# First heads of attention: the score row of head 0 copied straight from PSUM, head 2's q and k loaded into output buffers, two casts on ScalarE, and another order of work

## The chip, the core and the metric

The kernel runs on one NeuronCore of a Trainium2 chip. The metric is the device time of one execution in microseconds (us), the median of several runs. TensorE (PE) multiplies matrices, VectorE (DVE), ScalarE (ACT) and GpSimd (POOL) do the rest, and SyncE (SP) issues nearly all transfers (DMA) up to the last stage. The engines run on their own and wait for each other by semaphores that only count up.

## The reference

Three stages follow each other. Attention has 4 x 8 = 32 heads of 576 positions and width 64, with a mask in blocks of 64. Its output, 2304 tokens of width 512, goes through a gated MLP, and then each token goes to one of 8 experts.

```python
scores = scale * np.matmul(q, k.transpose(0, 1, 3, 2))
scores = np.where(block_i >= block_j, scores, -1000000000.0)
scores = scores - np.max(scores, axis=-1, keepdims=True)
attn = np.exp(scores)
attn = attn / (np.sum(attn, axis=-1, keepdims=True) + 1e-09)
x = np.matmul(attn, v)                  # 32 heads -> (4, 576, 512)
xk, xr = mix(x, x_prev, mu_k), mix(x, x_prev, mu_r)
x = sigmoid(xr @ w_r) * (np.maximum(xk @ w_k, 0.0) ** 2 @ w_v)
h = np.maximum(x[b, s] @ w1[e], 0.0)    # e: the token's expert, by its gate
out[b, s] = p[e] * (h @ w2[e])
```

## The kernel before

Attention takes one head after another, and the engines work on up to four heads at a time. For one head i the steps are these (the names are those in the code).

- SP loads q and k (`load_qk`, 576 KB) into one of two buffers `qk_raw[i % 2]`. ACT rounds the upper half into `aug` (`cast_tops`). DVE rounds everything into `hi` (`cast_hi`, a CAST of 128x1152) and writes the remainder of q into `aug` (`split_q_lo`). POOL then writes the remainder of k (`split_k`, L531), which waits for `q_split`. A next load into the same buffer waits for all three.
- PE makes rough scores (`head_max`, L707 and L710) in four groups, 0 to 3. DVE takes the negated maximum of each (`head_reduce`, L1380 for groups 0 to 2, L1383 for group 3). Group 3 reuses the banks of groups 0 and 1, so its products wait until DVE has read these.
- PE turns the five columns of maxima into a row (`head_row`, L718), DVE copies it (`copy_row`, L1391), and SP moves it by a transfer (`load_row`) into one partition of `aug`. There it is one row of the operand of the exact scores, so that the maximum is subtracted by the product.
- PE makes the exact scores (`head_scores`, L732 and L733, twelve products in five pieces), ACT takes their exponents (`head_exp`), and PE multiplies them by v. `head_pv_split` (L774 for the early half, L779 for the late) begins only when `row_copied` says that DVE has copied the row of the next head out of the same bank. `head_pv_late` (L787 to L789) adds the rounded part of the late half with the splits that DVE makes (`split_v`, L1483 and L1485, in even heads; `split_p`, L1491). ACT copies the result into `o_raw`, of which there are four buffers (`copy_out`).
- The sums of the exponents go by DMA to DVE (`invert`, L1396) and back, and POOL scales the output (`normalise`, L540).

From head 5 on DVE has one more piece of work in each head, the split of MLP weights (L1415).

The order on each engine is written out by hand. In the loop for head i, PE makes the scores of head i with the groups of `head_max(i + 2)` between them, and the row of head i + 1; DVE goes through this list:

```python
copy_row(i + 1); head_reduce(i + 2, 0); split_v(i // 2)        # split_v in even heads
split_wm_lo(i - 1 - WFIRST); cast_hi(i + NBUF); split_p(i)     # split_wm_lo from head 5
split_q_lo(i + NBUF); head_reduce(i + 2, 1); head_reduce(i + 2, 2)
invert(i - 1); head_reduce(i + 2, 3)
```

Before the loop stand the loads, the mask rows (built by DVE in `aug[0]` and copied to the other two `aug` by the transfers of `copy_masks`, which `aug_copied` counts), and the rough scores of heads 0 and 1.

Of the kernel before, what the change touches and what calls it, by code (L numbers as in the profile page):

```python
# [16 lines left out]
def attention_moe_program(nc, qkT, v, mu_k, mu_r, w_k, w_v, w_r, w_gate9, w1, w2, out):  # L17
# [36 lines left out]
    with ExitStack() as ctx:  # L54
# [258 lines left out]
        h_half, relu_half = sem("h_half"), sem("relu_half")  # L313
        pg_last, last_scaled, last_stored = [sem(n) for n in ("pg_last", "last_scaled", "last_stored")]
# [49 lines left out]
        SLOTS = NHEAD + NBUF  # L364
        out_rows = out.rearrange("b s d -> (b s) d")
# [3 lines left out]
        def _(sp):  # L369
            def load_qk(i):  # L370
                wait(sp, q_split, i - 1)
                wait(sp, k_split, i - 1)
                wait(sp, tops_cast, i - 1)
                sp.dma_start(qk_raw[:, i % 2, :, :],
                             qkT[i:i + 1].rearrange("a d w s -> (a d) w s")).then_inc(qk_loaded[i % 2], 16)
# [7 lines left out]
            def load_row(i):  # L383
# [3 lines left out]
                if i == 0:  # L387
                    sp.wait_ge(aug_copied, 16 * (NBUF - 1))
# [42 lines left out]
            load_qk(0)  # L431
            load_qk(1)
# [14 lines left out]
            for i in range(SLOTS):  # L447
# [6 lines left out]
                if i + 1 < NHEAD:  # L454
                    load_row(i + 1)
                if i + 4 < NHEAD:
                    load_qk(i + 4)
# [54 lines left out]
        def _(pool):  # L512
# [14 lines left out]
            def split_k(i):  # L527
# [3 lines left out]
                nc.gpsimd.tensor_tensor(hi[i % NBUF][DH:P, KEY, :], qk_raw[DH:P, i % 2, 1, :],  # L531
# [158 lines left out]
        def _(pe):  # L690
            mm = nc.tensor.matmul

            def head_max(i, groups):
# [4 lines left out]
                for g in groups:  # L698
                    if g == 0:
                        wait(pe, max_reduced, 4 * i)  # L700
                    if g == 3:
                        pe.wait_ge(max_reduced, 4 * i + 2)
                    for t in ((0, 1), (2,), (3,), (4,))[g]:
# [4 lines left out]
                        else:  # L708
                            for half in range(2):
                                last = mm(ps[0:TAIL, MAXB + half, 0:S // 2], q_tile,  # L710
# [8 lines left out]

            def head_scores(i, pieces):  # L720

                b = i % NBUF
                if pieces[0] == 0:
                    pe.wait_ge(k_split, i + 1)
                    pe.wait_ge(q_split, i + 1)
                    pe.wait_ge(row_loaded[i % 2], 16 * (i // 2) + 16)
# [422 lines left out]
        def _(act):  # L1149
# [19 lines left out]
            def copy_out(i, half):  # L1169
# [3 lines left out]
                if half == 0:  # L1173
                    wait(act, norm_done, i - NOUT + 1)
                nc.scalar.activation(o_raw[:, i % NOUT, q0:q1], ps[:, OUTB + half, 0:q1 - q0], ACT.Identity,
# [10 lines left out]
            def cast_tops(i):  # L1186

                wait(act, scores_t, 5 * (i - NBUF + 1))
                act.wait_ge(qk_loaded[i % 2], 16 * (i // 2) + 16)
                nc.scalar.activation(aug[i % NBUF][0:DH, 0:2 * S].rearrange("p (w s) -> p w s", w=2), qk_raw[0:DH, i % 2, :, :],  # L1190
                                     ACT.Copy).then_inc(tops_cast, 1)

            for i in range(NBUF):
                cast_tops(i)

# [24 lines left out]
            for i in range(NHEAD):  # L1220
                if i:
                    copy_out(i - 1, 1)
                head_exp(i)
# [691 lines left out]
```

## Time and profile before

| what | value |
|---|---|
| median of 3 runs | 771.11 us (770.67 to 771.77) |
| the profiled execution, its own time | 772.05 us |
| its span | 770.3 us |
| PE busy in the span | 741.0 us, 96% |
| DVE busy in the span | 494.1 us, 64% |

The span goes from the first to the last instruction. The share of busy time is a mean over stages: in attention, which ends at about 190 us of the span, DVE is nearly as busy as PE, and later it is not. Times in the rows are us from the span's start. A time line gives start, duration, engine, line, operation and operands, and in brackets how long the engine was idle before and what released it.

### The profile page before, as it was taken

How to read it: one execution, taken by the hardware profiler on the slowest of the kernel's cores; microseconds unless marked ns; L12 is line 12 of the kernel's file. 1: busy time of each engine (PE TensorE's matmuls, PEld its weight loads, DVE VectorE, ACT ScalarE, POOL GpSimd, SP SyncE). 2: the span in 40 equal slices, each digit the busy share in tenths (PEclk: the TensorE clock that was granted, in tenths of full speed). 3: DMA queues.
4: the chain of work that ended last, by engine and by line, in shares of the span. 5: the costliest groups of instructions: out<-in, count | busy, mean ns of one | idle time of the engine just before them, and what ended most of it. 6: DMA issues, size and time to landing. Idle time of an engine off the chain costs nothing.

```text
span 770.3 us, 13475 instructions
## 1 busy us (share of the span) xinstructions
PE 741.0 (96%) x4054; PEld 661.7 (86%) x4055; DVE 494.1 (64%) x905; ACT 357.5 (46%) x702; POOL 182.9 (24%) x215
## 2 busy tenths in 40 slices
PE   5999999998999999999999999999999999999994
PEld 4888888886989999999999998788888788888882
DVE  8899999996586856859487797622223745453261
ACT  4687877875652606244251432222124644353250
POOL 3345455453200000000020000223323232323231
PEclk9999999998999999999999999999999999999997
DMA  5667676551000010100101071167110176441000
GB/s 158 212 202 224 195 228 190 165 159 43 24 1 1 0 42 1 42 1 1 42 1 43 3 270 42 43 246 274 41 32 27 41 257 235 143 144 40 20 22 8
DMA packets 43063, 74.41 MB, mean 97 GB/s; under 512 B 10061, under 2 KB 20470, under 8 KB 43012
## 3 DMA queue, kind: packets, MB, share of 16 engines
q1 hardware_dynamic: 38676, 64.30, 25.3%
q0 software_dynamic: 4336, 9.47, 3.6%
q8 instruction: 27, 0.44, 0.2%
q14 instruction: 24, 0.20, 0.1%
HBM read 65.31 MB, written 10.57 MB: 99 GB/s over the span
## 4 chain that ended last, share of the span: by engine, by line
PE 83%; DVE 10%; issue 2%; ACT 2%; DMA 1%; ACTq 0%; POOL 0%; POOLq 0%; DVEq 0%
PE ps L841 20%; PE ps L842 20%; PE ps L843 20%; PE ps L779 3%; PE ps L707 2%; PE ps L999 2%; PE ps L733 2%; PE ps L732 2%; PE ps L831 2%; DVE negm L1380 2%; PE ps L710 2%; PE ps L774 1%; DVE sig L1564 1%; PE ps L753 1%; PE ps L908 1%
## 5 line engine op out<-in xcount | busy, mean ns | idle before, releaser
L841 PE MATMUL ps<-we_hi,hT_hi 128*128 (+1 forms) x176 | 73.4, 417 | 2.1 <-DVE o_sb L1856 1.4
L841 PE MATMUL ps<-we_hi,xgT_hi 128*128 (+1 forms) x176 | 70.6, 401 | 0.2 <-DVE xgT_lo L1755 0.2
L1317 ACT ACTIVATE hT_hi<-ps 128x512 fp32r<-128x512 f32 x44 | 26.1, 597 | 94.5 <-PE ps L999 49.4
L842 PE MATMUL ps<-we_lo,xgT_hi 128*128 (+1 forms) x176 | 69.7, 396 | 0.0
L843 PE MATMUL ps<-we_hi,xgT_lo 128*128 (+1 forms) x176 | 69.7, 396 | 0.0
L842 PE MATMUL ps<-we_lo,hT_hi 128*128 (+1 forms) x176 | 69.5, 395 | 0.0
L843 PE MATMUL ps<-we_hi,hT_lo 128*128 (+1 forms) x176 | 69.4, 394 | 0.0
L1151 ACT ACTIVATE pT<-ps 128x256 f32<-128x256 f32 (+2 forms) x192 | 63.1, 388 | 9.3 <-PE ps L733 8.9
L841 PE MATMUL ps<-xm_k_hi,wk_hi 128*128 128x384 f32 x192 | 65.2, 339 | 2.0 <-DVE ksq L1543 1.7
L841 PE MATMUL ps<-ksq_hi,wv_hi 128*128 128x384 f32 x192 | 66.0, 344 | 0.9 <-DVE yT L1578 0.9
L531 POOL TENSOR_TENSOR hi<-qk_raw,hi 64x576 fp32r<-64x576 f32 x32 | 45.2, 1412 | 85.8 <-DVE aug L1407 85.8
L842 PE MATMUL ps<-ksq_lo,wv_hi 128*128 128x384 f32 x192 | 64.9, 338 | 0.0
L843 PE MATMUL ps<-ksq_hi,wv_lo 128*128 128x384 f32 x192 | 64.9, 338 | 0.0
L843 PE MATMUL ps<-xm_k_hi,wk_lo 128*128 128x384 f32 x192 | 64.6, 336 | 0.0
L842 PE MATMUL ps<-xm_k_lo,wk_hi 128*128 128x384 f32 x192 | 64.5, 336 | 0.0
L1749 DVE TENSOR_TENSOR we_lo<-we_raw,we_hi (+1 forms) x48 | 55.6, 1221 | 11.3 <-ACT we_hi L1296 11.3
L1564 DVE RECIPROCAL sig<-sig 128x384 f32<-128x384 f32 x24 | 61.3, 2553 | 0.8
L1254 ACT ACTIVATE relu_k<-ps 128x384 f32<-128x384 f32 x48 | 23.6, 491 | 81.2 <-PE ps L843 81.2
L1762 DVE TENSOR_TENSOR hT_lo<-ps,hT_hi 128x512 fp32r<-128x512 f32 x44 | 30.0, 686 | 45.2 <-ACT hT_hi L1317 45.2
L1380 DVE TENSOR_REDUCE negm<-ps 128x1 fp32r<-128x128 f32 (+3 forms) x128 | 56.2, 479 | 2.1 <-PE ps L707 0.3
L732 PE MATMUL ps<-hi 128*128 128x256 f32 (+2 forms) x192 | 53.7, 297 | 2.3 <-ACT pT L1151 2.2
L628 POOL DMA_INDIRECT out<-o_sb,idx_out x21 | 21.5, 1023 | 139.4 <-DVE o_sb L1856 139.4
(277 smaller groups left out, 1835.4 us busy)
## 6 DMA issues: line engine op xcount, KB each, us to landing
we_raw<-w SPq DMA_DIRECT2D x12, 2048.0 KB, 11.8
qk_raw<-qkT SPq DMA_DIRECT2D x32, 576.0 KB, 3.9
v_sb<-v SPq DMA_DIRECT2D x16, 320.0 KB, 4.9
inv<-inv_scratch SPq DMA_DIRECT2D x32, 144.0 KB, 4.3
y_scratch<-ytok SPq DMA_DIRECT2D x6, 768.0 KB, 3.5
wk_raw<-w_k SPq DMA_DIRECT2D x8, 256.0 KB, 4.5
wv_raw<-w_v SPq DMA_DIRECT2D x8, 256.0 KB, 4.9
wr_raw<-w_r SPq DMA_DIRECT2D x4, 256.0 KB, 4.8
```

The source lines that it names most:

```text
L531: nc.gpsimd.tensor_tensor(hi[i % NBUF][DH:P, KEY, :], qk_raw[DH:P, i % 2, 1, :], hi[i % NBUF][DH:P, KEY, :].bitcast(F32), ALU.subtract).th ...
L732: mm(dst, hi[b][:, KEY, keys], hi[b][:, Q, q0:q1], start=True, stop=False)
L841: mm(dst, a_hi, b_hi, start=(k == 0), stop=False)
L842: mm(dst, a_hi, b_lo, start=False, stop=False)
L843: return mm(dst, a_lo, b_hi, start=False, stop=(k == n - 1))
L1151: return nc.scalar.activation(dst, src, ACT.Exp, **kw)
L1254: nc.scalar.activation(relu_k[:, f % 2, :], ps[:, KB + f % 2, 0:NT], ACT.Relu).then_inc(relu_done, 1)
L1317: nc.scalar.activation(hT_hi[:, half * FC // 2:(half + 1) * FC // 2, :].rearrange("p f t -> p (f t)"), ps[:, 3 + half, :], ACT.Copy).then_ ...
L1380: last = vec.tensor_reduce(negm[:, i % 2, t:t + 1], ps[:, bank, col:col + keys], AX.X, ALU.max, negate=True)
L1564: vec.reciprocal(sig[:, d, :], sig[:, d, :]).then_inc(sig_done, 1)
L1749: vec.tensor_tensor(we_lo[part][:, third], we_raw[part][:, third], we_hi[part][:, bass.ds(slot_at(j) + k * EPIECE, EPIECE)].bitcast(F32), ...
L1762: vec.tensor_tensor(hT_lo[:, fs, :].rearrange("p f t -> p (f t)"), ps[:, 3 + half, :], hT_hi[:, fs, :].rearrange("p f t -> p (f t)").bitca ...
```

## The change

It touches heads 0 to 4 only.

- **Row of head 0.** PE makes five products of one row each (`first_row`, 1x128) into one partition, and DVE copies them from PSUM into `aug[0]` (1x512 and 1x128). The transposing product, the copy into `m_rows` and the transfer are gone. The copies wait for `aug_copied`. Group 3 of head 0 goes to banks 0 and 1, so it no longer waits for DVE.
- **Head 2's q and k** go into `o_raw[:, 2:4]`, issued as the third transfer of the program, ahead of v and of the mask copies. Heads 3 and up use the two `qk_raw` buffers in turn, so heads 3 and 4 are loaded once heads 0 and 1 are done with them.
- **Casts.** `cast_hi` of heads 1 and 2 is an ACT instruction (128x1152) right behind `cast_tops`.
- **Order.** Head 0 is taken out of PE's and DVE's loops. PE makes all scores of head 0, the row of head 1, and then the v products with groups 0 to 2 of `head_max(2)` between them; group 3 comes last. DVE reduces all of head 2 and only then makes `cast_hi(3)` and `split_q_lo(3)`.

```diff
 def load_qk(i):
-    wait(sp, q_split, i - 1)          # and k_split, tops_cast
+    before = (0, 0, 0, 1, 2)[i] if i < 5 else i - 1
+    wait(sp, q_split, before)         # and k_split, tops_cast
...
-load_qk(0)
-load_qk(1)
+for i in range(NBUF):
+    load_qk(i)
 load_v(0)
 for b in range(1, NBUF):
     copy_masks(b)
-load_qk(2)
-load_row(0)
 load_qk(3)
+load_qk(4)
+load_row(1)
...
 # TensorE
+def first_row(ts):
+    pe.wait_ge(max_reduced, 3 if ts[0] == 0 else 4)
+    for t in ts:
+        last = mm(ps[0:1, OUTB + t // 4, t % 4 * P:(t % 4 + 1) * P], negm[:, 0, t:t + 1], ident_r[:, :],
+                  start=(t % 4 == 0), stop=(t in (3, 4)))
+    last.then_inc(first_row_out, 1)
...
 head_max(0, (0, 1, 2, 3))
-head_row(0)
+first_row((0, 1, 2, 3))
+first_row((4,))
 pe.wait_ge(aug_copied, 16 * (NBUF - 1))
 head_max(1, (0, 1, 2, 3))
-for i in range(NHEAD):
+head_scores(0, (0, 1, 2, 3, 4))
+head_row(1)
+head_pv_split(0, (0, 1))
+head_max(2, (0, 1, 2))
+head_pv_split(0, (2, 3, 4, 5))
+head_pv_late(0)
+head_max(2, (3,))
+for i in range(1, NHEAD):
...
 # ScalarE
 for i in range(NBUF):
     cast_tops(i)
+    if i:
+        nc.scalar.activation(hi[i][:, :, :], raw_of(i), ACT.Copy).then_inc(hi_cast_act, 1)
...
 # VectorE
-copy_row(0)
-cast_hi(1)
+dve.wait_ge(aug_copied, 16 * (NBUF - 1))
+dve.wait_ge(first_row_out, 1)
+first = aug[0][DH:DH + 1, QLO:QLO + CH * P]
+vec.tensor_copy(first[:, 0:4 * P], ps[0:1, OUTB, :])
+dve.wait_ge(first_row_out, 2)
+vec.tensor_copy(first[:, 4 * P:CH * P], ps[0:1, OUTB + 1, 0:P]).then_inc(row_copied, 1)
 split_q_lo(1)
 for g in range(4):
     head_reduce(1, g)
-cast_hi(2)
-split_q_lo(2)
...
 for i in range(NHEAD):
     if i + 1 < NHEAD:
         copy_row(i + 1)
+    if i == 0:
+        split_q_lo(2)
+        split_v(0)
+        split_p(0)
+        for g in range(4):
+            head_reduce(2, g)
+        cast_hi(NBUF)
+        split_q_lo(NBUF)
+        continue
     if i + 2 < NHEAD:
         head_reduce(i + 2, 0)
```

On DVE, this stood before between the row copy of head 0 and that of head 2 (`hi_72` is head 1's buffer, `hi_68` head 2's, `hi_70` head 3's):

```order
L1391 CAST m_rows<-ps 5x128
L1402 CAST hi_72<-qk_raw 128x1152
L1407 TENSOR_TENSOR aug_73<-qk_raw,hi_72 64x576
L1380 TENSOR_REDUCE negm<-ps 128x1 x4
L1383 TENSOR_REDUCE negm<-ps 64x1
L1402 CAST hi_68<-qk_raw 128x1152
L1407 TENSOR_TENSOR aug_69<-qk_raw,hi_68 64x576
L1391 CAST m_rows<-ps 5x128
L1380 TENSOR_REDUCE negm<-ps 128x1 x2
L1483 CAST v_hi<-v_sb 128x128
```

And this stands in the changed kernel from the row copy of head 1 (first row) to that of head 2 (last row):

```order
L1440 CAST m_rows<-ps 5x128
L1459 TENSOR_TENSOR aug_69<-o_raw,hi_68 64x576
L1537 CAST v_hi<-v_sb 128x128
L1539 TENSOR_TENSOR v_lo<-v_sb,v_hi 128x128
L1545 TENSOR_TENSOR pT_lo<-pT,p_hi 128x320
L1428 TENSOR_REDUCE negm<-ps 128x1 x4
L1432 TENSOR_REDUCE negm<-ps 64x1
L1451 CAST hi_70<-qk_raw 128x1152
L1459 TENSOR_TENSOR aug_71<-qk_raw,hi_70 64x576
L1440 CAST m_rows<-ps 5x128
```

The two casts of heads 1 and 2 are gone from DVE, and head 3's cast and split (`hi_70`, `aug_71`), which stood ahead of the last three reductions of head 2, stand behind all five, directly ahead of head 2's row copy.

On PE, this followed the scores of head 0 before (L774 and L779 are its v products, `aug_69` is head 2):

```order
L707 MATMUL ps<-aug_69 128x384
L774 MATMUL ps<-pT,v_sb 128x256
L774 MATMUL ps<-pT,v_sb 128x128
L707 MATMUL ps<-aug_69 128x512
L779 MATMUL ps<-pT,v_sb 128x320 x2
L779 MATMUL ps<-pT,v_sb 128x192
L779 MATMUL ps<-pT,v_sb 128x64
L710 MATMUL ps<-aug_69 64x288 x2
L787 MATMUL ps<-p_hi,v_hi 128x320
```

And this follows them in the changed kernel:

```order
L738 MATMUL ps<-ident_r,negm 5x128
L805 MATMUL ps<-pT,v_sb 128x256
L805 MATMUL ps<-pT,v_sb 128x128
L727 MATMUL ps<-aug_69 128x128
L727 MATMUL ps<-aug_69 128x256
L727 MATMUL ps<-aug_69 128x384
L727 MATMUL ps<-aug_69 128x512
L810 MATMUL ps<-pT,v_sb 128x320 x2
```

The row of head 1 (the first row) now stands directly ahead of the v products that wait for its copy, and groups 0 and 1 of head 2 have moved behind them; the two 64x288 products of group 3 now follow the last v product.

## Rows read from the trace of the kernel before

**Rows 1.** The page, part 1: busy time of each engine in the span.

```profile
PE 741.0 (96%) x4054; PEld 661.7 (86%) x4055; DVE 494.1 (64%) x905; ACT 357.5 (46%) x702; POOL 182.9 (24%) x215
```

**Rows 2.** One stretch of attention: PE, PEld, DVE, ACT, POOL busy, clock, DMA, GB/s.

```profile
60.00:100.00 40.00, 39.38 (x244) 34.74 (x244) 37.11 (x88) 31.86 (x80) 20.56 (x15) 1.00 0.69 212
```

**Rows 3.** The chain that ended last, 0 to 60 us: start, us, piece.

```profile
13.13 0.21 PE ps L732
...
16.54 0.11 PE ps L733
...
17.13 1.28 PE ps L774 x4
...
18.68 1.57 PE ps L779 x8
20.25 0.27 PE ps L710 x2
...
20.96 0.12 PE ps L732
...
23.19 0.66 PE ps L774 x4
...
26.36 0.12 PE ps L732
```

**Rows 4.** The same chain from 60 to 195 us, its pieces on DVE.

```profile
60.55 0.41 DVE negm L1380
...
71.69 0.42 DVE negm L1380
```

**Rows 5.** Time line of all engines, 0 to 26 us.

```profile
8.31 0.34 SPq L374 DMA_DIRECT2D qk_raw<-qkT  x1
8.49 0.75 DVE L1383 TENSOR_REDUCE negm<-ps 64x1 fp32r<-64x576 f32 x1 [0.24 <-PE ps L710]
...
9.81 0.74 DVE L1402 CAST hi<-qk_raw 128x1152 fp32r<-128x1152 f32 x1
...
10.58 0.75 DVE L1407 TENSOR_TENSOR aug<-qk_raw,hi 64x576 fp32r<-64x576 f32 x1
11.26 1.67 DVE L1380 TENSOR_REDUCE negm<-ps 128x1 fp32r<-128x128 f32 x4
...
12.04 1.16 ACT L1190 ACTIVATE aug<-qk_raw 64x1152 fp32r<-64x1152 f32 x1 [4.73 <-DMA qk_raw<-qkT]
...
15.53 1.40 POOL L531 TENSOR_TENSOR hi<-qk_raw,hi 64x576 fp32r<-64x576 f32 x1 [2.64 <-DVE aug L1407]
...
16.02 1.00 DVE L1483 CAST v_hi<-v_sb 128x128 fp32r<-128x128 f32 x1
...
20.55 0.75 DVE L1383 TENSOR_REDUCE negm<-ps 64x1 fp32r<-64x576 f32 x1 [0.42 <-PE ps L710]
...
21.62 0.28 DVE L1391 CAST m_rows<-ps 5x128 fp32r<-5x128 f32 x1 [0.32 <-PE ps L718]
...
22.97 0.76 DVE L1402 CAST hi<-qk_raw 128x1152 fp32r<-128x1152 f32 x1 [0.38 <-PE ps L733]
```

**Rows 6.** Time line of DVE, 19 to 62 us.

```profile
27.90 0.22 DVE L1483 CAST v_hi<-v_sb 128x128 fp32r<-128x128 f32 x1
...
36.94 0.21 DVE L1396 RECIPROCAL sums<-sums 64x9 f32<-64x9 f32 x1 [0.30 <-DMA sums<-o_raw]
```

**Rows 7.** DVE's groups, 0 to 190 us: busy, mean ns, idle before, its releasers.

```profile
L1402 DVE CAST hi<-qk_raw 128x1152 fp32r<-128x1152 f32 x32 | 24.1, 752 | 0.8 <-PE ps L733 0.8
...
L1391 DVE CAST m_rows<-ps 5x128 fp32r<-5x128 f32 x32 | 8.9, 278 | 10.2 <-PE ps L718 10.2
```

**Rows 8.** Stretches of 1 us: clock, mean share of the 16 DMA engines, GB/s.

```profile
3.00:4.00 1.00, 1.00 0.99 392
...
7.00:8.00 1.00, 1.00 0.28 36
```

**Rows 9.** Waits of SP's queue, 0 to 30 us: what for, total, times, longest.

```profile
SPq L388 <- DMA aug<-aug: 0.6, 1, 0.6
```

More of the change, by code:

```diff
@@ L364, in attention_moe_program, with raw_of, raw_in, rows_in @@
         SLOTS = NHEAD + NBUF
+        def raw_of(i):
+            if i == 2:
+                return o_raw[:, 2:4, :]
+            return qk_raw[:, i if i < 2 else (i - 1) % 2, :, :]
+        def raw_in(i):
+            if i < 2:
+                return qk_loaded[i], 16
+            if i == 2:
+                return qk_loaded_2, 16
+            return qk_loaded[(i - 1) % 2], 16 * ((i + 1) // 2)
+        def rows_in(i):
+            return 16 * ((i + 1) // 2)
         out_rows = out.rearrange("b s d -> (b s) d")
@@ L370, in load_qk @@
             def load_qk(i):
-                wait(sp, q_split, i - 1)
[L372 to L375, printed above, removed]
+                before = (0, 0, 0, 1, 2)[i] if i < 5 else i - 1
+                wait(sp, q_split, before)
+                wait(sp, k_split, before)
+                wait(sp, tops_cast, before)
+                sp.dma_start(raw_of(i), qkT[i:i + 1].rearrange("a d w s -> (a d) w s")).then_inc(raw_in(i)[0], 16)
             def load_v(j):
@@ L453, in _ @@
                     spread_sums(i - 1)
-                if i + 1 < NHEAD:
+                if 1 < i + 1 < NHEAD and i:
                     load_row(i + 1)
-                if i + 4 < NHEAD:
+                if i and i + 4 < NHEAD:
                     load_qk(i + 4)
@@ L700, in head_max @@
                         wait(pe, max_reduced, 4 * i)
-                    if g == 3:
+                    if g == 3 and i:
                         pe.wait_ge(max_reduced, 4 * i + 2)
@@ L709, in head_max @@
                             for half in range(2):
-                                last = mm(ps[0:TAIL, MAXB + half, 0:S // 2], q_tile,
+                                last = mm(ps[0:TAIL, MAXB + half if i else PBANK[half], 0:S // 2], q_tile,
                                           a[:, KHI + half * (S // 2):KHI + (half + 1) * (S // 2)], start=True, stop=True)
@@ L725, in head_scores @@
                     pe.wait_ge(q_split, i + 1)
-                    pe.wait_ge(row_loaded[i % 2], 16 * (i // 2) + 16)
+                    if i:
+                        pe.wait_ge(row_loaded[i % 2], rows_in(i))
+                    else:
+                        pe.wait_ge(row_copied, 1)
                 for j in pieces:
@@ L1375, in head_reduce @@
                 if g == 0:
-                    wait(dve, max_row, i - 1)
+                    wait(dve, max_row, i - 2)
                 for t in ((0, 1), (2,), (3,), (4,))[g]:
```

39 lines of the change are left out of this document (26 added, 13 removed).

## The prediction

> **What bounds the kernel now.** I read four views, from coarse to fine. The page comes first: PE is busy 96% of the span and DVE 64% [rows 1]. The reader is to see that the second figure misleads, since it is a mean over stages. So I took a stretch of attention next: in 40 us there PE is busy 39.38 and DVE 37.11 [rows 2]. Both are full, and neither can make up much time. Third, the chain that ended last. From 13.13 us on it runs on PE alone for a long time; the scores of head 1 begin at 20.96 and those of head 2 at 26.36, so a head costs 5.40 us, all of it PE [rows 3]. Later the chain crosses to DVE once in two heads: its pieces begin at 60.55 and 71.69, which is 11.14 us for a pair, or 5.57 a head [rows 4]. Fourth, what DVE idles for in attention: 10.2 us ahead of the row copies, 0.32 in each of nearly all heads, which is the way from the last reduction over PE's row product back to DVE, and 0.8 us in all ahead of 32 casts, two waits of 0.4 [rows 5, 7]. So DVE's list is a loop without slack too, apart from heads 1 and 3, where those two waits are. What follows: a delay of DVE or PE at head 2 is carried to the end of attention, and every later stage starts from there. The start decides, and I work out when each engine gets to the copy of head 2's row, which DVE begins at 21.62 now [rows 5].
>
> One more thing about the start: TensorE is slow there. The same four v products take 1.28 us at 17.13 and 0.66 at 23.19, and the eight after 18.68 take 1.57 [rows 3], which for 896 columns in four passes is the upper level of 2.4 GHz, while the first is the lower, 1.2 GHz. So the clock rises at about 18.5 us, after the chain has run on PE without a break from 13.13. The column of the granted clock says 1.00 before that as well [rows 8], so the durations are the evidence.
>
> **The change, part by part.**
>
> *Row of head 0.* The last reduction of head 0 ends at 9.24, and the split of head 1, L1407, starts at 10.58, behind the row copy and the cast of head 1 (0.74) [rows 5]. Now the cast is ScalarE's. ACT has 4.73 us idle before 12.04, and a cast of 1152 columns takes it 1.16 [rows 5]: two of these fit, and that the work moves costs nothing. DVE's two new copies: 1x128 about 0.25 (the row copy, 0.28), 1x512 about 0.6, between 0.54 and 0.7 by the reductions of that width, since four of these with 1280 columns take 1.67 [rows 5]. Group 3 starts 0.2 sooner, as its 0.24 of idle time goes [rows 5]. With no other wait DVE would be at L1407 at 9.05 + 0.05 + 0.6 + 0.25 = 9.95, a gain of 0.6.
>
> *But the copies wait for the mask rows.* SP's queue issued at 8.31, was done at 8.65 and then waited 0.6 for `aug_copied`, so these landed at 9.25 [rows 5, 9]. Now 576 KB more stand ahead of them, 1.5 us at 392 GB/s [rows 8]. The DMA engines were only 0.28 busy from 7 to 8 us [rows 8], so the mask copies did not wait for data to the end and some of the 1.5 is absorbed. I take 0.5: landing at 9.8, bounds 9.25 and 10.75. Then the copies end at 10.65 and L1407 starts at 10.6, against 10.58. The gain of 0.6 is gone (bounds: 0.55 gained to 0.9 lost). The transfer removed saves nothing in itself: before, the scores of head 0 at 13.13 came straight behind the rough scores of head 1, not behind a landing.
>
> *PE, head 0.* Scores begin at 13.15. Their twelve products, whose first and last piece are at 13.13 and 16.54, add up to 2.77 us on the chain without the other products between them [rows 3] (3200 columns at 1.2 GHz are 2.67), so they end at 15.9. The row product of head 1 ends at 16.05, DVE copies from 16.25 to 16.53 (0.3 for the way there, 0.28) [rows 5], and the v products, which wait for `row_copied`, begin at 16.57: PE idles 0.5 where it had other work before. Early v products 1.28, to 17.85 [rows 3]. Groups 0 to 2 of head 2 are 1280 columns, 1.07 at the lower level; 0.65 of it before 18.5 and 0.3 behind, to 18.8. Late v products 1.57, to 20.4, and the three behind them 0.44 (from 20.52, where L710 ends, to 20.96) [rows 3], to 20.82. Only now come the products of group 3, which stood at 20.25.
>
> *DVE, head 0 to 2.* From 16.53 it has `split_q_lo(2)` (0.75), the splits of v (0.5) and p (0.5) and the reductions of groups 0 to 2 (1.7, the length of four such ones) [rows 5]: it is done at about 20.0 and then waits for group 3. The reduction started 0.30 after the product (20.55) [rows 3, 5]: now 21.11 to 21.86. Behind it stand now the cast and split of head 3, 0.68 and 0.68 from start to start (9.81, 10.58 less idle, 11.26) [rows 5]. So the row of head 2 is copied at 21.11 + 0.68 + 0.68 + 0.68 = 23.15, not 21.62: **1.53 late**. PE is ahead of that; it has to wait for `row_copied` at its v products of head 1.
>
> *Head 1.* DVE does not have to wait 0.38 for PE ahead of its cast [rows 5], as PE has the scores done by 23.2: -0.38. But that cast meets POOL. `split_k(3)` starts 0.17 behind L1407's end, at 23.4, and runs 1.40 to 24.8; the cast of head 4 wants to start at 24.05. Before, the cast L1483 began at 16.02 under a POOL instruction of 15.53 to 16.93 and took 1.00, and at 27.90 beside no such one 0.22 [rows 5, 6]: 0.77 more with 0.91 of POOL's left. With 0.75 left I take +0.6, bounds 0 and 0.75. The Trainium skill (SBUF — State Buffer, section "SBUF: two separate sides") says that a VectorE copy in a two-port mode and a GpSimd instruction share a port pair by an exclusive lock, and the later one stands still until the earlier is through; the row of 1.00 us agrees, and by the rule the sum would have 0.75 in the place of 0.6. The same lock holds, it says, for VectorE instructions with two SBUF inputs beside a GpSimd one that reads SBUF; by that the splits of v and p of head 0 would stand behind `split_k(2)`, which the idle time ahead of group 3 takes up but for 0.3 at most, and no row here shows that pair.
>
> *Heads 2 to 6.* POOL's split comes 1.9 late with the rest, so the load of head 5's q and k is issued at about 24.9, not 23.0; its cast on DVE stands at 29.7, and the issue-to-use time of 4.8 covers it. At 36.94 DVE waited 0.30 for the sums' transfer [rows 6]; that transfer is itself later with PE's products, so I credit 0.1. The row product of each head had up to 0.2 between the end of the last reduction and PE's arrival; I credit 0.1.
>
> *Sum:* 1.53 - 0.38 + 0.6 - 0.1 - 0.1 = **+1.55 us**. The profiled execution took 772.05 us by its own time and 770.3 in its span, so 773.6 and 771.85; the median shown is 0.94 below it, so 771.11 + 1.55 = 772.7. About 0.2% (1.5 us) is what a measurement of this kernel can tell from no change, and my number lies right at it.
>
> **Rivals.**
>
> - *The row waits little and POOL costs nothing.* Mask rows land at 9.25, POOL does not hold up the cast, and more of the sums' wait is absorbed (0.28): 1.53 - 0.2 - 0.38 - 0.28 - 0.1 = +0.6, so 771.7. For it: engines had DMA time to spare at 7 us. Against: the row of 1.00 us. No change that can be told, 0.20.
> - *The clock rises later.* PE's new idle 0.5 us falls just before the old rise. If that delays the rise until past 21.9, the late v and the three late products (2.0 us at the upper level) and half of the groups take double: +1.9 at group 3, so 1.55 + 1.8 = +3.3, 774.4. For it: before, the rise came only after unbroken work. 0.18. The Trainium skill (TensorE: Matmul & The Clock Gate, "Part 1: The HAM clock gate") has the slow clock as the resting state that activity lifts, at a moment that varies from run to run; the one rise in this trace agrees with the first, and no run here shows the second.
> - *The clock rises earlier,* as PE is now unbroken from 13.15 to 16.05 with scores only. If it rose by 15.1, PE would be at group 3 at about 19.4, 1.4 sooner, and DVE at the row at 21.8: 1.55 - 1.3 = +0.25, 771.4. 0.06.
> - *The other side: the head start is kept.* DVE does two casts fewer (1.5 us) and 0.6 more of copies. If what I call a loop had slack, DVE would catch up, and what would remain is PE's lead. For it to decide, the row of head 2 must not be copied later than 21.1: group 3 would have to be reduced by 19.1, which is before PE, with the same products to make as before and 0.5 of idle time, can get there. Worth at best the 0.6 of DVE's lead plus the 0.75 that L1483 lost to POOL and the 0.38 ahead of the cast: -1.7, 769.4. 0.05.
>
> **How the numbers follow.** The forecast case (head 2's row 1.2 to 1.9 late, POOL's hold in part or whole, together +1.0 to +2.2) has 0.48, of which I put 0.28 above the bound of 1.5 and 0.20 below, because POOL's hold has more room upwards. Slower by over 0.2%: 0.28 + 0.18 (late clock) = 0.46, and 0.01 for the rest. Within 0.2%: 0.20 + 0.20 + 0.06 = 0.46. Faster: 0.05 and 0.02 for what I have not thought of. The range runs from 770.9, below the early clock's 771.4, to 774.5, which holds about half of the late clock's case: it leaves out 0.07 below and 0.09 above.
>
> **What the profile after would show.** The first row's copies on DVE starting at about 9.8, held by DMA, not at 9.05. ACT with its two casts of 128x1152 done by 10.7. Head 0's scores at about 13.1. PE idle 0.5 ahead of the first v product. DVE idle about 1 us ahead of the reduction of group 3 of head 2 at 21.1, then the row copied at about 23.15. The cast of head 4, at 24, stretched to 1.3 us. PE idle about 1 us ahead of group 3 of head 3, released by DVE. From head 3 on the same list as before at a constant distance of about 1.6. Wrong would be: a distance that shrinks over the heads (then there is slack), a rise of the clock elsewhere than at 18.5 (the v products at 16.6 and 18.8 tell), or a start of head 1's scores before 20.5.

## The result: 2.5 us slower, and the profile after

| what | kernel before | changed kernel |
|---|---|---|
| median of 20 runs each | 771.80 us (769.46 to 773.27) | 774.29 us (771.87 to 776.34) |
| ratio, with its 95% interval | | 1.0031 (1.0020 to 1.0042), that is 1.5 to 3.2 us |
| the profiled executions, own time | 772.05 us | 771.90 us |
| head 2's row copied by DVE | 21.62 | 24.61 |
| head 6's row copied | 43.47 | 46.25 |

The change costs 2.5 us. The forecast was 1.55 with a range up to 3.4 above, so the sign and the range held, and the size was too small. In plain times 774.29 lies 0.2 below the upper end of the range, 774.5. The page of the changed kernel differs from [rows 1] by nothing that tells of it:

```profile
PE 740.0 (96%) x4058; PEld 660.7 (86%) x4059; DVE 494.5 (64%) x904; ACT 359.9 (47%) x704; POOL 182.9 (24%) x215
```

The profiled executions of the two kernels even took the same time, though the changed one is 2.8 us behind all through attention. The stretches of 5 us behind attention say why: TensorE's granted clock fell there in the kernel before (first two rows, columns as in [rows 2]), and in the changed kernel it did not (last two rows). A level of 0.50 is 1.2 GHz and 1.00 is 2.4 GHz.

```profile
185.00:190.00 5.00, 4.13 (x13) 3.50 (x14) 1.76 (x5) 2.99 (x10) 0.00 (x0) 0.56 0.14 33
190.00:195.00 5.00, 5.00 (x23) 3.93 (x22) 0.00 (x0) 3.54 (x10) 1.40 (x1) 0.75 0.01 0
```

```profile
185.00:190.00 5.00, 2.83 (x20) 2.30 (x19) 2.98 (x5) 3.16 (x10) 1.39 (x1) 1.00 0.03 4
190.00:195.00 5.00, 5.00 (x29) 4.05 (x28) 1.80 (x6) 4.06 (x11) 1.41 (x1) 1.00 0.15 32
```

Such a fall, at 185 to 190 us, stands in 9 of the 14 traces of this study, of both orders. What 0.56 and 0.75 leave out of twice 5 us is 2.2 + 1.25 = 3.45 us of full speed, of which PE, busy for 9.13 of the 10, lost about 3 (an estimate from these rows). One pair of profiles would have told "no change". The mean granted clock, which is on record for each execution, bears this out. The changed kernel's 20 executions fall into two groups: eight with a mean of 0.996 or more took 771.87 to 772.89 us, and twelve below it 774.08 to 776.34; the profiled one is of the first group and the second fastest of all. The profiled execution of the kernel before (mean 0.991) is slower than its median. So I compare when each engine gets to the same work in attention, and leave the end of the span to the medians.

This is the chain of the changed kernel from 6 to 29 us: start, duration, piece.

```profile
6.06 4.05 DMA aug<-aug
10.13 0.68 DVE aug L1503
...
11.04 0.75 DVE aug L1459
...
13.59 0.21 PE ps L763
...
16.47 0.42 issue
16.89 1.62 PE ps L805 x4
18.51 1.17 PE ps L727 x4
19.68 1.99 PE ps L810 x8
...
22.17 0.28 PE ps L730 x2
22.51 0.64 issue
23.15 0.75 DVE hi L1451
...
25.41 1.47 DVE hi L1451
...
28.46 0.48 PE ps L730 x2
```

A piece called issue is time for which the chain names no releaser: by the time line, at 16.47 it is PE's wait for the row copy and at 22.51 the reduction of group 3 itself. Before, this chain was on PE alone from 13.13 on [rows 3]. Now it comes from the mask rows' transfer, has PE standing still for 0.42 ahead of the first v product (L805), and leaves PE for DVE twice: behind group 3 of head 2 (L730), and for the cast of head 4. (That cast has two rows in the chain: L1451 at 23.15 is head 3's and at 25.41 head 4's.) The time line of the same stretch:

```profile
9.43 1.15 ACT L1239 ACTIVATE hi<-o_raw 128x1152 fp32r<-128x1152 f32 x1
10.13 0.68 DVE L1503 CAST aug<-ps 1x512 fp32r<-1x512 f32 x1 [1.21 <-DMA aug<-aug]
...
16.50 0.28 DVE L1440 CAST m_rows<-ps 5x128 fp32r<-5x128 f32 x1 [2.13 <-PE ps L738]
...
17.61 1.56 POOL L551 TENSOR_TENSOR hi<-o_raw,hi 64x576 fp32r<-64x576 f32 x1 [4.26 <-DVE aug L1459]
17.62 0.29 DVE L1539 TENSOR_TENSOR v_lo<-v_sb,v_hi 128x128 fp32r<-128x128 f32 x1
17.83 1.70 DVE L1545 TENSOR_TENSOR pT_lo<-pT,p_hi 128x320 fp32r<-128x320 f32 x1
...
22.48 0.75 DVE L1432 TENSOR_REDUCE negm<-ps 64x1 fp32r<-64x576 f32 x1 [1.36 <-PE ps L730]
...
24.61 0.27 DVE L1440 CAST m_rows<-ps 5x128 fp32r<-5x128 f32 x1
...
24.85 1.40 POOL L551 TENSOR_TENSOR hi<-qk_raw,hi 64x576 fp32r<-64x576 f32 x1 [2.90 <-DVE aug L1459]
...
25.34 1.54 DVE L1451 CAST hi<-qk_raw 128x1152 fp32r<-128x1152 f32 x1
26.80 0.48 DVE L1545 TENSOR_TENSOR pT_lo<-pT,p_hi 128x320 fp32r<-128x320 f32 x1
...
30.05 0.28 DVE L1440 CAST m_rows<-ps 5x128 fp32r<-5x128 f32 x1 [0.32 <-PE ps L738]
```

Nearly every step of the prediction can be found: the copies held by the masks' transfer, the idle PE, DVE waiting 1.36 for group 3, the row of head 2 copied behind the cast and split of head 3, and the cast of head 4 stretched under POOL's split. The row copies follow those of before by 2.99 (head 2), 3.03, 3.04, and then 2.78 us from head 5 to the end of attention. The chain's pieces on DVE show the same distance in the place of [rows 4]:

```profile
63.34 0.41 DVE negm L1428
...
74.47 0.41 DVE negm L1428
```

Again 11.13 for a pair of heads, now 2.79 later.

### The profile page after: what moved, and what is told of

Its sections match the earlier page's. It is cut to its first block, busy times and chain, and to the rows that moved or that the text cites. A ratio compares the mean times of both kernels' runs of the same rounds, so it can differ in the third digit from the quotient of the medians.

```text
span 770.2 us, 13482 instructions
## 1 busy us (share of the span) xinstructions
PE 740.0 (96%) x4058; PEld 660.7 (86%) x4059; DVE 494.5 (64%) x904; ACT 359.9 (47%) x704; POOL 182.9 (24%) x215
## 4 chain that ended last, share of the span: by engine, by line
PE 83%; DVE 10%; issue 2%; ACT 2%; DMA 1%; ACTq 0%; POOL 0%; POOLq 0%; SPq 0%; DVEq 0%
PE ps L881 20%; PE ps L883 20%; PE ps L882 20%; PE ps L810 3%; PE ps L727 2%; PE ps L1039 2%; PE ps L764 2%; PE ps L763 2%; PE ps L871 2%; DVE negm L1428 2%; PE ps L730 1%; PE ps L805 1%; DVE sig L1627 1%; DVE hi L1451 1%; PE ps L948 1%
## 5 line engine op out<-in xcount | busy, mean ns | idle before, releaser
L551 POOL TENSOR_TENSOR hi<-qk_raw,hi 64x576 fp32r<-64x576 f32 x31 | 43.8, 1411 | 83.0 <-DVE aug L1459 83.0
L648 POOL DMA_INDIRECT out<-o_sb,idx_out x21 | 21.5, 1023 | 139.4 <-DVE o_sb L1919 139.4
```

Of the source, the lines that this page charges most:

```text
L551: nc.gpsimd.tensor_tensor(hi[i % NBUF][DH:P, KEY, :], raw_of(i)[DH:P, 1, :], hi[i % NBUF][DH:P, KEY, :].bitcast(F32), ALU.subtract).then_i ...
```

## The experiments

Thirteen kernels were compared with the kernel before, always on the same chip. Of each I give the ratio, and two moments from its trace: when the clock rose (from where the records of the granted clock begin; the durations agree) and when the rows of heads 2 and 6 were copied. The first four ask for the place of the delay, the next four for the parts, the last four for the clock.

| kernel | clock rises | row of head 2 | row of head 6 | ratio (95% interval) |
|---|---|---|---|---|
| before | 18.37 | 21.62 | 43.47 | 1 |
| changed | 20.41 | 24.61 | 46.25 | 1.0031 (1.0020, 1.0042) |
| masks_first | 19.88 | 24.12 | 45.87 | 1.0039 (1.0025, 1.0053) |
| cast_before_g3 | 21.61 | 24.07 | 45.66 | 1.0035 (1.0022, 1.0048) |
| g3_before_late | 22.96 | 25.39 | 47.01 | 1.0049 (1.0036, 1.0063) |
| before_delay | 19.27 | 23.19 | 44.01 | 1.0008 (0.9993, 1.0022) |
| fill_gap | 19.46 | 23.73 | 45.36 | 1.0029 (1.0019, 1.0040) |
| old_order | 20.98 | 22.91 | 44.82 | 1.0013 (0.9994, 1.0032) |
| row_only | 21.81 | 23.49 | 45.09 | 1.0002 (0.9992, 1.0012) |
| mended | 19.16 | 23.15 | 44.94 | 1.0017 (1.0008, 1.0026) |
| before_warm | 6.46, falls 9.88, 20.12 | 22.32 | 43.94 | 0.9997 (0.9986, 1.0007) |
| after_warm | 5.62, falls 9.04, 22.69 | 25.71 | 47.34 | 1.0014 (1.0000, 1.0029) |
| old_order_warm | 4.53, falls 7.94, 18.18 | 21.49 | 43.43 | 1.0006 (0.9995, 1.0017) |
| before_warmer | 6.22, stays | 20.60 | 42.17 | 0.9978 (0.9964, 0.9992) |

**masks_first: head 2's load behind the mask copies.**

```diff
-            for i in range(NBUF):
-                load_qk(i)
+            load_qk(0)
+            load_qk(1)
...
+            load_qk(2)
```

> The changed kernel with the load of head 2's q and k issued behind v and the mask copies instead of ahead of them. Marks: the landing of the mask rows (10.1 us in the changed kernel, 9.25 before), the copy of head 2's row on VectorE (24.61 against 21.62) and that of head 6's row (46.25 against 43.47). If the load ahead of the masks is what holds up the first copies: masks at 9.3, the first copy of the row at 9.3, scores of head 0 at 12.8 instead of 13.6, and head 6's row at 45.5 to 45.9, less if the clock rises sooner as well. If the mask rows were late for another reason: nothing moves. If only the moment of the clock's rise counts (20.4 us in the changed kernel, 18.4 before): head 6's row moves only as far as that moment does, by half of it or less.

```profile
9.71 0.68 DVE L1504 CAST aug<-ps 1x512 fp32r<-1x512 f32 x1 [0.79 <-DMA aug<-aug]
```

The copies start 0.42 earlier, head 1's row 0.42 and head 2's 0.49. The wait for the masks is real, and it is a small part: 0.38 us at head 6, with a rise of the clock 0.53 earlier, to which the reckoning below puts all but 0.1 of it. The median, 774.16, does not show it. The masks landed at 9.7 and not at 9.3 as expected (9.25 before); what held them for the other 0.4 is not shown.

**cast_before_g3: the cast and split of head 3 ahead of the last reduction of head 2 on DVE.**

```diff
-                    for g in range(4):
+                    for g in range(3):
                         head_reduce(2, g)
                     cast_hi(NBUF)
                     split_q_lo(NBUF)
+                    head_reduce(2, 3)
```

> The changed kernel with one edit on VectorE: the cast and the q split of head 3 stand ahead of the last reduction of head 2 (group 3), in the 1.36 us that it waits there for TensorE. If the order of VectorE's list makes the lateness: head 2's row is copied at 23.5 instead of 24.61, the cast of head 4 no longer meets the GpSimd split of head 3 (0.75 instead of 1.54 us), head 6's row at 45.1 instead of 46.25, and the median about 1.1 us below the changed kernel's. If the late clock is the cause, TensorE is what is waited for, VectorE's order gives nothing: head 6's row at 46.2.

```profile
20.91 0.74 DVE L1451 CAST hi<-qk_raw 128x1152 fp32r<-128x1152 f32 x1
...
23.00 0.75 DVE L1432 TENSOR_REDUCE negm<-ps 64x1 fp32r<-64x576 f32 x1 [0.56 <-PE ps L730]
...
25.42 0.76 DVE L1451 CAST hi<-qk_raw 128x1152 fp32r<-128x1152 f32 x1 [0.39 <-PE ps L764]
```

Two things go at once: the cast and split fill DVE's wait for group 3 (1.36 becomes 0.56), and the cast of head 4 takes 0.76 again, since POOL's split of head 3 is over by then. The row of head 6 is 0.59 earlier although the clock rose 1.20 later; 1.15 earlier was expected. The ratio, 1.0035, is no lower than the changed kernel's. All eight executions of this kernel had a mean clock below 0.996. Beside the eight of masks_first that had one too, on the same chip, their median is 1.0 lower (773.33 against 774.32), which is the size of the gain in the rows.

**g3_before_late: the products of group 3 ahead of the three late v products.**

```diff
-            head_pv_late(0)
             head_max(2, (3,))
+            head_pv_late(0)
```

> The changed kernel with one edit on TensorE: the two products of group 3 of head 2 stand ahead of the three late v products of head 0 instead of behind them. By the order theory the reduction starts 0.45 sooner (22.0), head 2's row is copied at 24.15 and head 6's at 45.8. By the rival, that VectorE is held by something else at that place (the GpSimd lock on the p split, which took 1.70 us), nothing moves: 24.6 and 46.25.

DVE waited 2.08 for group 3 in place of 1.36, with the clock risen 2.55 later than in the changed kernel. The edit moves these products ahead of 0.44 us of others, and the clock takes more than that away. The run decides nothing on the edit: neither of the two expectations, 45.8 and 46.25 for head 6's row, was met (47.01). It was the first to show how far the moment of the rise wanders.

**before_delay: a reduction of 1.60 us ahead of the row copy of head 2, in the kernel before.** Its result is used by nobody.

```diff
+                if i == 1:
+                    vec.tensor_reduce(idle_out[:, :], ident.unsqueeze(1).to_broadcast([P, 11, P]), AX.XY, ALU.max)
                 if i + 1 < NHEAD:
                     copy_row(i + 1)
```

> The kernel before with one dummy reduction of about 1.5 us on VectorE ahead of the copy of head 2's row (its result is never read). It asks whether anything behind takes up a delay there. No slack: head 2's row at 23.1, head 6's at 44.6 (1.5 less the 0.3 that the wait for the sums' transfer takes up), the same distance at head 30, and a time 1.1 to 1.3 us above the kernel before. Slack, so that the head start rival could have held: head 6's row back at 43.5 to 43.8 and no change in time.

```profile
20.99 0.75 DVE L1384 TENSOR_REDUCE negm<-ps 64x1 fp32r<-64x576 f32 x1 [0.84 <-PE ps L711]
21.66 1.60 DVE L1497 TENSOR_REDUCE idle_out<-idw 128x1 f32<-128x1408 f32 x1
23.19 0.27 DVE L1392 CAST m_rows<-ps 5x128 fp32r<-5x128 f32 x1
...
23.91 0.74 DVE L1403 CAST hi<-qk_raw 128x1152 fp32r<-128x1152 f32 x1
```

Row copies of heads 2, 3, 4 and 6 were late by 1.57, 0.82, 0.82 and 0.54, and this stayed to the end of attention. Of the 1.57, PE made 0.44: group 3 was reduced at 20.99 and not 20.55, with a rise 0.90 later. Head 6's row at 44.01 is neither the 44.6 of no slack nor the 43.5 to 43.8 of full slack. So a delay at head 2 is not carried whole: DVE's round for head 1 takes up 0.75 of it and that for head 3 0.27, and from then on nothing is given back. I had counted 0.38 and 0.1 for these. The rows show where most of the rest was: in the kernel before DVE needs 1.35 from the row copy (21.62) to its next cast (22.97) [rows 5], here 0.72, since PE has everything ready. The median moved by 0.3, within what can be told from nothing.

**fill_gap: groups 0 and 1 of head 2 between head 1's row and the first v product.**

```diff
             head_row(1)
+            head_max(2, (0, 1))
             head_pv_split(0, (0, 1))
-            head_max(2, (0, 1, 2))
+            head_max(2, (2,))
```

> The changed kernel with one edit on TensorE: groups 0 and 1 of head 2 (640 columns, 0.55 us at the lower clock) stand between the row product of head 1 and the first v product, where TensorE idled 0.4 us for the row's copy. In the four traces with that gap the clock rose at 19.9, 20.4, 21.6 and 23.0 us, in the two with the start of before, which has no gap, at 18.4 and 19.3. If the gap is what puts the rise off: no idle time at 16.5, a rise before 20.2, head 2's row copied at 22.8 to 24.0 (24.61 in the changed kernel), head 6's at 45.6 or less, and a median 1 us or more below the changed kernel's, since its later runs had the rise later than its profiled one. If the moment of the rise is drawn freely: 19.9 to 23 again, head 6's row near 46.2.

```profile
16.33 0.85 PE ps L727 x3
17.19 1.28 PE ps L805 x4
18.47 0.43 PE ps L727
```

The idle time is gone, and something else with it: the four v products take 1.28 here, as before the change [rows 3], and 1.62 where they follow the idle stretch (the changed kernel, masks_first, cast_before_g3, g3_before_late, after_warm). The chain counts a piece from the end of the one before it. In the time line the four last 1.48 behind other work and 1.62 behind the stop, so 0.20 of the 0.34 is the start of the first product, which otherwise runs beside the end of the product before. PE's stop costs 0.42 and then 0.34 in the chain. Head 6's row is 0.89 earlier; the clock rose 0.95 earlier. The median was expected 1 us or more below the changed kernel's and is not: the ratio is 1.0029 beside 1.0031.

**old_order: all parts of the change, with the order of before on PE, DVE and ACT, and the masks first.**

```diff
...
-            head_scores(0, (0, 1, 2, 3, 4))
-            head_row(1)
-            head_pv_split(0, (0, 1))
-            head_max(2, (0, 1, 2))
-            head_pv_split(0, (2, 3, 4, 5))
-            head_pv_late(0)
-            head_max(2, (3,))
-            for i in range(1, NHEAD):
+            for i in range(NHEAD):
...
-                if i == 0:
-                    split_q_lo(2)
-                    split_v(0)
-                    split_p(0)
-                    for g in range(4):
-                        head_reduce(2, g)
-                    cast_hi(NBUF)
-                    split_q_lo(NBUF)
-                    continue
...
```

> The changed kernel's parts without its order: head 0's row by one-row products, head 2's q and k in output buffers (loaded behind the mask copies), the casts of heads 1 and 2 on ScalarE, but TensorE's and VectorE's lists in the order of before. If the new order is what costs: head 0's scores at 12.8 (13.1 before), head 2's row at 20.8 to 21.3 (21.62 before), head 6's at 42.6 to 43.3 (43.47), the median 0.2 to 0.8 us below the kernel before. If the parts themselves cost (the copies of the first row, the casts on ScalarE): head 6's row later than 43.6.

```profile
21.84 0.75 DVE L1422 TENSOR_REDUCE negm<-ps 64x1 fp32r<-64x576 f32 x1 [2.25 <-PE ps L731]
```

DVE waits 2.25 for group 3, where it waited 0.42 before [rows 5]. It is ready at 19.59, where it was at 20.13 before: the parts do save it 0.54, and PE, with its clock up only at 20.98, takes all of it. So the rows expected of the order (20.8 to 21.3 and 42.6 to 43.3) were missed by 1.5 us or more, and the median is not below the kernel before. The ratio cannot be told from 1, but its interval reaches the changed kernel's 1.0031 too; what tells the two orders apart are the rows at one clock, below.

**row_only: only the row of head 0 by one-row products, in the kernel before.** The edit is the first one of the change, with group 3 of head 0 in other banks.

> The kernel before with the first part alone: head 0's row by five one-row products and two copies, no transfer, and group 3 of head 0 in the free banks. The two copies (0.68 and 0.27) take the place of one of 0.28 and wait for the mask rows, which land at 9.25. So the cast of head 1 starts at 10.2 instead of 9.81, and everything is 0.3 to 0.4 late: head 2's row at 21.9, head 6's at 43.8, the time the same or 0.3 above. By the rival, that the transfer was on the path: head 0's scores before 12.9 and head 6's row before 43.3.

The row's two copies start at 9.24 and take 0.61 and 0.30 from start to start; behind them stands DVE's cast of head 1, at 10.15, where it began at 9.81 [rows 5]. The way over the transfer was hidden, and the copies cost DVE 0.34 more. DVE waited 1.92 for group 3 at head 2, with a rise at 21.81: PE bounds here too. Because of this rise the rows of heads 2 and 6, expected at 21.9 and 43.8, came at 23.49 and 45.09; the ratio, 1.0002, is as expected.

**mended: masks first, the gap filled and the cast ahead of group 3, in the changed kernel.** It joins the three edits above.

> The changed kernel with three edits together: mask copies ahead of head 2's load, groups 0 and 1 of head 2 in TensorE's gap, and the cast and split of head 3 ahead of the last reduction of head 2. If these three places make the lateness: masks at 9.3, no gap, no wait of VectorE over 0.6 us ahead of group 3, head 4's cast 0.75 us; head 2's row at 21.7 to 22.7, head 6's at 43.6 to 44.4, the median within 1 us of the kernel before. If something else in the new order costs: head 6's row above 45.

```profile
17.42 1.70 DVE L1547 TENSOR_TENSOR pT_lo<-pT,p_hi 128x320 fp32r<-128x320 f32 x1
...
20.64 0.74 DVE L1453 CAST hi<-qk_raw 128x1152 fp32r<-128x1152 f32 x1
...
22.09 0.74 DVE L1434 TENSOR_REDUCE negm<-ps 64x1 fp32r<-64x576 f32 x1
```

It takes off about half of the loss (772.58 against 771.16 for the kernel before), not all. The rows missed what was expected: head 2's 23.15 (21.7 to 22.7), head 6's 44.94 (43.6 to 44.4), just under the 45 that would have spoken for something else in the order. Now the last reduction has no idle time ahead of it: DVE bounds, and its list holds the splitting of p at 1.70 instead of 0.48, under POOL's split of head 2. That hold sat in DVE's wait for group 3 before; with the cast moved there it is on the path. This hold, of about 1.2 us, was not in the expectation.

**before_warm, after_warm, old_order_warm: the clock out of the comparison?** Twelve fp32 products of 128x128 that nobody reads were added on PE where it waits.

```diff
+            warm(9)
...
             head_max(0, (0, 1, 2, 3))
...
-            head_max(1, (0, 1, 2, 3))
+            head_max(1, (0, 1, 2))
+            warm(3)
+            head_max(1, (3,))
```

> The kernel before with 12 extra fp32 products of 128x128 on TensorE, whose result nobody reads: 9 ahead of the first rough scores, where TensorE waits for head 0's transfer anyway, and 3 ahead of the products of group 3 of head 1, where it waits for VectorE. They add nothing to what is computed. They are to take TensorE's clock out of the comparison of the three kernels of this call. Theory (the order sets most of the lateness, the clock the rest): with the clock risen by 9 to 13 us the row of head 2 is copied at about 21.1 instead of 21.62, head 6's at about 43.0, and the median is 0.5 to 1.5 below the kernel before. Rival (the products do not move the rise, or it falls back in TensorE's idle stretch at 11 to 12.4): rise at 18 to 23 us as in the other runs, and the median of the kernel before.

> The same 12 extra products in the changed kernel. Theory (order): the clock risen early for both, head 2's row at about 22.0 and head 6's 0.9 to 1.2 after that of the kernel before with the same products; the median 0.8 to 1.5 above it. Rival (the lateness is the clock's alone): head 6's row within 0.3 of the kernel before with the same products, and medians within 0.4 of each other. Second rival (POOL's hold and the serial tail behind group 3 of head 2 count in full whatever TensorE does): 2.0 or more above.

> The same 12 extra products in the kernel with the changed parts (row of head 0 by one-row products, head 2 in output buffers, two casts on ScalarE), head 2's load behind the mask copies and the order of before on all engines. Theory (TensorE at its lower clock bounds the start, and hides what the parts save): with the clock up early the parts show, head 2's row at 20.3 to 20.6, head 6's at about 42.5, and the median is the lowest of the three, 0.3 to 0.8 below the kernel before with the same products. Rival (the parts save nothing in any case): within 0.2 of the kernel before with the same products.

The rival won in its second form: the clock rose at once and fell back, in all three. In stretches of before_warm:

```profile
5.00:8.00 3.00, 2.25 (x10) 1.55 (x9) 2.93 (x7) 1.79 (x2) 1.16 (x1) 1.00 0.57 148
8.00:10.00 2.00, 1.16 (x7) 0.82 (x6) 1.68 (x4) 0.00 (x0) 0.23 (x1) 0.97 0.32 61
10.00:14.00 4.00, 3.49 (x15) 2.80 (x14) 3.73 (x8) 1.73 (x3) 1.39 (x1) 0.50 0.42 133
14.00:20.00 6.00, 6.00 (x20) 5.05 (x21) 5.77 (x12) 3.33 (x8) 2.65 (x3) 0.50 0.66 197
```

PE had little to do around 8 us (busy for 1.16 of 2), the clock fell at 9.88, and then it was at 0.50 through 6 us of unbroken work. So the three kernels were again compared at different clocks. Yet they give what was missing, two traces of one order at different rises. old_order copies head 6's row at 44.82 with a rise at 20.98 and at 43.43 with one at 18.18: 0.50 us for each us. The changed kernel (46.25 and 47.34, rises at 20.41 and 22.69) gives 0.48, the kernel before (43.47 and 43.94, 18.37 and 20.12) only 0.27. And old_order_warm against the kernel before, with nearly the same rise (18.18 and 18.37), stands at 21.49 against 21.62 and 43.43 against 43.47. With PE at the lower clock the parts of the change bring nothing. The medians are 770.98, 772.17 and 771.91 us, against 771.46 for the kernel before: the changed kernel is 1.2 above before_warm, and old_order_warm, which was expected lowest, is not.

**before_warmer: 19 such products in the kernel before,** 5 of them between 6.6 and 9 us.

```diff
+            warm(9)
...
-            head_max(0, (0, 1, 2, 3))
+            head_max(0, (0, 1, 2))
+            warm(2)
+            head_max(0, (3,))
+            warm(3)
             head_row(0)
...
-            head_max(1, (0, 1, 2, 3))
+            head_max(1, (0, 1, 2))
+            warm(5)
+            head_max(1, (3,))
```

> The kernel before with 19 extra products instead of 12: 9 ahead of the first rough scores, 2 ahead of the products of group 3 of head 0, 3 ahead of its row product and 5 ahead of group 3 of head 1, so that TensorE has little idle time between 6.5 us and the scores of head 0. With 12 the clock had risen at 6.46 and fallen back at 9.88, behind the idle stretch from 7 to 9 us. Theory (the start is bound by TensorE at its lower clock, and the fall came from that idle stretch): the granted clock stays at 1.00 through 13 us and beyond, the v products of head 0 take 0.66 instead of 1.28, VectorE bounds the start, head 2's row is copied at 20.6 to 21.1 and head 6's at 42.5 to 43.0, and the median is 0.3 to 1.0 below the kernel before. Rival 1 (the clock falls whatever these products do): as with 12 products, head 6's row at 43.5 to 44.2 and no difference in the median. Rival 2 (the clock stays up at the start, but what is won is lost at a later fall, as near 190 us): the rows early, the median not below.

```profile
5.00:8.00 3.00, 2.53 (x14) 2.18 (x14) 2.93 (x7) 1.69 (x2) 1.17 (x1) 1.00 0.59 153
8.00:10.00 2.00, 1.82 (x13) 1.45 (x12) 1.68 (x4) 0.00 (x0) 0.23 (x1) 1.00 0.33 78
10.00:14.00 4.00, 2.91 (x22) 2.44 (x21) 3.96 (x8) 1.75 (x3) 1.40 (x1) 1.00 0.38 123
14.00:20.00 6.00, 4.76 (x29) 4.09 (x28) 5.94 (x12) 3.09 (x8) 3.44 (x3) 1.00 0.69 195
```

```profile
19.02 0.48 PE L710 MATMUL ps<-aug 69*64 69x288 f32 x2 [1.24 <-DVE negm L1392]
```

```profile
18.42 1.14 DVE L1392 TENSOR_REDUCE negm<-ps 128x1 fp32r<-128x384 f32 x2
19.53 0.75 DVE L1395 TENSOR_REDUCE negm<-ps 64x1 fp32r<-64x576 f32 x1
20.60 0.28 DVE L1403 CAST m_rows<-ps 5x128 fp32r<-5x128 f32 x1 [0.32 <-PE ps L718]
```

The clock stays at 1.00 although PE is busy for only 2.91 of the 4 us from 10 on. DVE is busy all the time (5.94 of 6), has no wait ahead of group 3, and PE waits 1.24 for it: the bound of the start has changed sides. Head 2's row is 1.02 earlier, head 6's 1.30, more than expected (42.5 to 43.0; it is 42.17). The median is 768.96 (12 runs, 767.38 to 771.0) against 771.19 for the kernel before on the same chip (17 runs), ratio 0.9978 (0.9964 to 0.9992). This is the version that beats both. The start explains 1.30 of the 2.2 us; that the other 0.9 comes from fewer falls of the clock near 190 us fits this trace, which has none. The mean clocks on record agree: 5 of its 12 executions had 0.996 or more, against 3 of the 17 of the kernel before, and inside the two groups it is 1.0 (767.76 against 768.81) and 0.8 us (770.73 against 771.50) faster. Where the clock fell in those executions is not on record.

## Why the prediction was right, and where it was too small

Its sign, its mechanism and its range held; the size of the first term did not: head 2's row is 2.99 late, not 1.53. At head 6 the terms missed by +1.46 (head 2), -0.18 (head 1) and -0.06 (later heads), which takes 1.55 to 2.8. Two of the signs that the prediction itself called wrong came: the clock rose elsewhere than at 18.5, and the distance shrank, by 0.26 behind head 4.

**The lag of head 2's row** was built up over four numbers. The mask rows landed at 10.1, not 9.8, which made L1459 start at 11.04 and not at 10.6, and of this 0.32 reached the first v product (16.89, not 16.57). Those products took 1.62 and not 1.28, the 0.34 that fill_gap lays to the idle time ahead of them; I had priced the stop itself and not the start behind it. And the clock rose at 20.41, not at 18.5, so that groups 0 to 2 took 1.17 (I had 0.95, and of that 0.3 should have been 0.21, the 0.42 left of the 1.07 at twice the clock) and the late v products 1.99 (1.57). Together group 3 came at 22.17 instead of 20.82, 1.35 late, and the rest of DVE's steps took 2.44 where I had 2.33. Piece by piece the masks and the restart have 0.66 of this and the clock 0.70 (0.22, 0.42 and 0.06 in the last three products); by the slope of 0.50 the clock has 0.95. The shares depend on the order of reckoning, since work that moves behind the rise gets cheaper; the total does not.

**At one clock** the forecast was nearer. A slope of 0.50 takes the kernel before from 43.47 to 44.49 for a rise at 20.41, and the changed kernel is at 46.25: the order costs 1.76. In the same way masks_first gives 1.65 and after_warm 1.71. The forecast was 1.55. With the kernel before's own slope, 0.27, it is 2.2, so the order costs about 1.8 to 2.2. The kernels with the order of before have nothing left to explain at 0.50: old_order 0.05, row_only -0.10. cast_before_g3 gives 0.57 by this reckoning, so about 1.2 us of the order's cost is one decision, the cast and split of head 3 behind the last reduction; this difference needs only the slope of the changed order. One slope for kernels of both orders is an assumption, and it holds only where PE bounds: mended has that edit and two more and comes out at 1.08, above 0.57, since there DVE bounds and a later clock would cost less.

**Head 1** came out nearly right in sum (+0.04, forecast +0.22) by two errors that cancel. PE's being ahead gave back 0.75 where I had 0.38 (before_delay: 1.57 to 0.82); POOL's hold cost 0.79 where I took 0.6 (the cast took 1.54, and 0.75 without POOL). POOL's hold on the split of p (1.70 for 0.48), which the prediction named and left to DVE's idle time, did stay in it here: DVE still waited 1.36.

**The slack of the later heads** was 0.26 in the changed kernel (3.04 to 2.78), 0.2 in my sum, and from head 5 on no distance changed by more than 0.2 in any kernel, where the prediction had a constant one.

**The rivals.** "Little wait" is out: the masks landed late and POOL held the cast. "The head start is kept" is out, and old_order shows why even the old order does not keep it: PE bounds the start. "The clock rises later" came half true, 2 us later instead of 3.4. Whether PE's idle 0.42 does this, as I had feared, stays open. The five traces with the idle stretch rose at 19.88 to 22.96 (mean 21.5), the nine without at 18.18 to 21.81 where they rose late at all (eight, mean 19.7; the ninth is before_warmer). The means differ by less than the members of either group, with one trace for each kernel. Dealt at random, the thirteen values would give so large a difference about 2 times in 100, so the tendency is there, but the kernels differ in more than this stop. If it does, it would help to explain why the medians of the changed order are high.

**The start's true bound** was named and not followed up. The prediction read off the durations that PE ran at 1.2 GHz until 18.5, took that as given, and put DVE's list beside it as the other full engine. DVE had 0.42 of slack there only because PE was slow, and with the clock up, DVE is the one that bounds.

## What to carry to other kernels

Before shortening the list of one engine at a start, look whether TensorE is at its lower clock there: old_order took 0.54 us from VectorE and row_only put 0.34 on it, and neither moved the median clear of the kernel before, while 19 products for nothing won 1.3 us in attention and 2.2 in the median. Work that can be done while another engine is awaited belongs ahead of the wait: one cast and one split on the wrong side of a reduction cost about 1.2 us by the rows (1.0 between executions of like clock) and put the next cast under GpSimd. Once they are moved, the next hold shows, as the split of p in mended. And where two kernels differ by 0.3%, one profile of each can show the opposite of the medians; compare the same step of both, at the same clock.

## What the runs showed of the hardware

- The moment at which TensorE's clock rises for good at the start lay between 18.18 and 22.96 us in 13 traces, all with nearly unbroken work from 13 us on, and each us of it cost 0.50, 0.48 and 0.27 us at head 6 in the three pairs of traces of one order. Without the added products the record begins with that rise, and the column of the granted clock says 1.00 ahead of it, while durations are those of 1.2 GHz (1.28 for four products that take 0.66 later). The Trainium skill (TensorE: Matmul & The Clock Gate, "Part 1: The HAM clock gate") gives the moment of the rise a spread of 0.5 us either way from run to run; here, over different kernels, with one trace of each, the moments lie 4.8 us apart; the spread of one kernel was not traced.
- Raised early, it fell back at 9.88 where PE was busy for 1.16 of the 2 us from 8 on (before_warm), and stayed up where PE was busy for 1.82 of them (before_warmer).
- A splitting of p on VectorE with two inputs in SBUF (128x320) took 1.70 beside a GpSimd instruction that had begun 0.22 before it, and 0.48 alone. The prediction had a rule for that pair that no row had shown (the Trainium skill, SBUF — State Buffer, section "SBUF: two separate sides": an exclusive lock for the whole instruction). The row of p agrees: GpSimd's instruction ended at 19.17, and the split at 19.53, 0.36 behind. The split of v, also with two inputs in SBUF, began 0.01 behind the same GpSimd instruction and took 0.29, as at other times, so that row shows no lock; the starts may be too close to tell which came first.
- Behind 0.42 us of idle time four products of TensorE at the lower clock took 1.62 in the chain against 1.28 behind other work, in five traces; in the time line it is 1.62 against 1.48, and the rest is the start that no longer runs beside the product before.
